# Query groups 0 and 1 loaded in 128-byte runs and transposed by VectorE, like the other 22

## The chip, the cores and the metric

One core of a Trainium2 chip runs the whole kernel. The metric is the time of one execution on the device in microseconds (us); of two kernels the one with the lower median is faster.

The engines run side by side, each through its own list of instructions in order, and wait for one another on semaphores: TensorE (PE in the profile, its weight loads PEld), VectorE (DVE), ScalarE (ACT), GpSimd (POOL) and SyncE (SP, which here only issues loads and stores). 16 DMA engines carry these out.

## What is computed

Attention of 12288 queries over 768 keys, whose result goes through two small networks. All is float32.

```python
kv_pool = kv.reshape(B, H // 4, 4, W // 4, 4, C).mean(axis=(2, 4))   # 384 x 32 pixels of 128 -> 768 keys
k = v = kv_pool.reshape(B, -1, C) @ w_sr
s = (q @ k.transpose(0, 2, 1)) / np.sqrt(C)                          # q: 12288 x 128
a = np.exp(s - s.max(-1, keepdims=True))
a /= a.sum(-1, keepdims=True) + 1e-09
x = a @ v                                                            # 12288 x 128
h = x @ w_in;  x = (np.maximum(h, 0) + alpha * np.minimum(h, 0)) @ w_out      # 128 -> 2048 -> 128
h = x @ w_in2
g = (a0 + a1*h + a2*h**2 + a3*h**3) / (1 + abs(b0)*abs(h) + abs(b1)*h**2 + 1e-06)
out = g @ w_out2                                                     # 2048 -> 128
```

Each row of q gives one row of out, so rows may be taken in any order, if the output is written back in the same.

## The kernel before

**Stages.** The kernel has three. At the start (0 to 27 us) kv is loaded in six chunks of 1 MB (each 128 rows of 8 KB), pooled 4 x 4 into 128 keys a chunk, and multiplied by w_sr to k and v. Then comes attention over 24 groups of 512 queries (to about 290 us), and then both networks over the same 24 groups (to 1530 us).

**Precision.** TensorE multiplies in a fast float32 form (fp32r). To keep precision an operand is split in two: its high part, rounded by ScalarE as it is written (k_hi, q_hi, x_hi), and its low part, the difference (k_lo, q_lo, x_lo). split_product adds three products of such parts.

**The start in the order of each engine.** SyncE issues all loads on one queue: chunk 0 in two halves, chunk 1, query group 0, chunk 2, query group 1, chunks 3 and 4, chunk 5 in two halves, w_in1, w_out1, the coefficients (L207 to L218), and then query groups 2 and later, each as soon as its buffer is free (L219 to L232). Chunk c is pooled in four units of 512 columns. VectorE sums two or three of them (pool_keys, L949), TensorE multiplies the others directly with a matrix that adds rows (pooled_transpose, L1429), and then VectorE's sums too (L1433). ScalarE copies the result out (copy_pooled_t, L463), and TensorE multiplies it by w_sr (key_chunk, L1442), after every third chunk to values as well (L1446). ScalarE and VectorE split k and v (keys_hi, keys_lo, values_hi, values_lo). TensorE takes its steps in the order pooled_transpose(0), (1), key_chunk(0), queries(0), pooled_transpose(2), key_chunk(1), queries(1), and so on (L1514 to L1525). VectorE has query_lo(0) behind pool_keys(2) and query_lo(1) behind pool_keys(3) (L1041 to L1044). ScalarE has query_hi(0) ahead of copy_pooled_t(2), and query_hi(1) ahead of copy_pooled_t(3) and keys_hi(0) (L533 to L544).

**Query groups 0 and 1.** q_in (the same memory as neg_part, 128 x 2 x 512, one buffer for even and one for odd groups) is loaded with one transfer for each: partition p takes rows 4p to 4p + 3 of its group, 2 KB in one run. Scores need queries with their 128 components over the partitions. So TensorE transposes four 128 x 128 tiles into PSUM bank Q_T (queries, L1474), ScalarE rounds from there (query_hi, L502), and VectorE subtracts (query_lo, L989).

**Query groups 2 to 23.** Four transfers load a group, one for each quarter j of the components: partitions 32j to 32j + 31, rows of 32 floats (128 bytes) each, 512 runs a transfer (L225). One 32 x 32-block transpose by VectorE (turn_query, L996) then gives q_turned with the components over the partitions; ScalarE rounds it, and GpSimd subtracts (query_lo, L264). This leaves the queries of a group in another order, and the stores undo it: four transfers of 512-byte runs for a group (L239), where groups 0 and 1 have one of 2 KB runs (L236).

**Memory.** early is a name for the memory that x_hi and x_lo take later: kv_in lies in the half of x_lo, and q_turned is before the change the last 1024 columns of it, where chunk 5 of kv lies at the start.

**Behind the start.** TensorE's first score product waits for k_lo (both halves) and q_lo (tile_scores, L1478). From then on the steps of all engines are written out by hand, without a branch.

Of the kernel before, what the change touches and what calls it, by code (L numbers as in the profile page):

```python
# [7 lines left out]
F32 = mybir.dt.float32  # L8
# [5 lines left out]
P = 128  # L14
# [20 lines left out]
def build(nc, q, kv, w_sr, w_in1, w_out1, alpha, w_in2, w_out2, coef_p, coef_q, out):  # L35
# [15 lines left out]
    q_groups = q[0].rearrange("(g p t) c -> g p (t c)", p=P, t=TILES)  # L51
    q_parts = q[0].rearrange("(g a n) (j b) -> g j a n b", a=SIDE, n=GROUP // SIDE, b=SIDE)
    out_groups = out.rearrange("(g p t) c -> g p (t c)", p=P, t=TILES)
# [3 lines left out]
    with ctx:  # L57
# [53 lines left out]
        q_turned = early[:, 2 * tokens - 2 * GROUP:].rearrange("p (b n) -> p b n", b=2)  # L111
# [10 lines left out]
        Q_T, P_T, ATT = 4, (5, 6, 4), 7  # L122
# [4 lines left out]
        for name in (  # L127

            *(f"ld_kv{c}" for c in range(CHUNKS)), "ld_kv_first", "ld_kv_rest", "spread0", "row_sums_done", "ld_wsr", "ld_in1", "ld_out1", "ld_in2", "ld_out2", "ld_al", "ld_ab", "ld_q0", "ld_q1", "ld_turned0", "ld_turned1", "q_turned", "q_lo_pool", "st_out",
# [5 lines left out]
            "qt_ready", "q_hi_done", "q_lo_done", "s_ready", "max_done", "shift_done", "exp_done", "eps_done", "inv_done",  # L135
# [15 lines left out]
        def stores(g):  # L151
            return g + (P // SIDE - 1) * max(g - 2, 0)
# [51 lines left out]
        def _(sp):  # L204

            half = UNITS // 2 * POOL_SIDE * P
            sp.dma_start(kv_in[:, 0, 0:half], kv_rows[0, 0, :, 0:half]).then_inc(s["ld_kv0"], 16)  # L207
            sp.dma_start(kv_in[:, 0, half:], kv_rows[0, 0, :, half:]).then_inc(s["ld_kv_first"], 16)
            for c in range(1, CHUNKS - 1):
                sp.dma_start(kv_in[:, c, :], kv_rows[c // 2, c % 2]).then_inc(s[f"ld_kv{c}"], 16)  # L210
                if c <= 2:
                    sp.dma_start(q_in[:, c - 1, :], q_groups[c - 1]).then_inc(s[f"ld_q{c - 1}"], 16)
# [6 lines left out]
            for g in range(GROUPS - 2):  # L219
                if g < 2:  # L220
                    sp.wait_ge(s["qt_ready"], g + 1)
                else:
                    sp.wait_ge(s["q_turned"], g - 1)
                for j in range(P // SIDE):
                    sp.dma_start(q_in[j * SIDE:(j + 1) * SIDE, g % 2, :].rearrange("a (n b) -> a n b", b=SIDE),  # L225
                                 q_parts[g + 2, j]).then_inc(s[f"ld_turned{g % 2}"], 16)
# [6 lines left out]
            for g in range(GROUPS):  # L233
                sp.wait_ge(s["y2_out_done"], g + 1)
                if g < 2:
                    sp.dma_start(out_groups[g], y_out[:]).then_inc(s["st_out"], 16)  # L236
                else:
                    for r in range(P // SIDE):
                        sp.dma_start(out_parts[g, r], y_out[r * SIDE:(r + 1) * SIDE, :].rearrange("a (t c) -> a t c", t=TILES)).then_inc(s["st_out"], 16)  # L239
# [4 lines left out]
        def _(pool):  # L244
# [16 lines left out]
            def query_lo(g):  # L261
                if group(g):
                    pool.wait_ge(s["q_hi_done"], g + 1)
                    nc.gpsimd.tensor_tensor(q_lo[:, g % 2, :], q_turned[:, g % 2, :], q_hi[:, g % 2, :].bitcast(F32),  # L264
                                            ALU.subtract).then_inc(s["q_lo_pool"], 1)
# [16 lines left out]

            for g in range(STEPS):
# [170 lines left out]
        def _(act):  # L454
# [38 lines left out]
            def query_hi(g):  # L493
                if group(g):
                    if g < 2:
                        act.wait_ge(s["qt_ready"], g + 1)
                        turned = banks[:, Q_T, :]
                    else:
                        act.wait_ge(s["q_turned"], g - 1)
                        turned = q_turned[:, g % 2, :]  # L500
                    after(act, s["s_ready"], (g - 1) * TILES)
                    nc.scalar.activation(q_hi[:, g % 2, :], turned, ACT.Copy).then_inc(s["q_hi_done"], 1)  # L502
# [436 lines left out]
        def _(dve):  # L939
# [46 lines left out]
            def query_lo(g):  # L986
                if group(g):
                    dve.wait_ge(s["q_hi_done"], g + 1)
                    nc.vector.tensor_tensor(q_lo[:, g % 2, :], banks[:, Q_T, :], q_hi[:, g % 2, :].bitcast(F32),  # L989
                                            ALU.subtract).then_inc(s["q_lo_done"], 1)  # L990

            def turn_query(g):
                if group(g):
                    dve.wait_ge(s[f"ld_turned{g % 2}"], 16 * (P // SIDE) * (g // 2))
# [850 lines left out]
```

## Time and profile before

| | us |
|---|---|
| median of 3 runs | 1532.26 (1532.25 to 1532.49) |
| profiled execution | 1533.03 |
| its span, first to last instruction | 1530.6 |

| engine | busy, us | share of the span | instructions |
|---|---|---|---|
| TensorE, matmuls | 1497.5 | 98% | 8181 |
| VectorE | 1434.1 | 94% | 2269 |
| ScalarE | 1402.4 | 92% | 2714 |
| GpSimd | 1259.0 | 82% | 1369 |

All but the first 27 us are filled almost without a gap on TensorE. These shares are means over the whole span; the start looks otherwise, and the rows below are mostly from there. A busy matmul row overlaps the next, so that 98% is no measure of TensorE at its peak. In lists by time, a row can stand for several instructions of one kind (x16), and in brackets is how long the engine had been idle before and what released it. The rows of SPq are issues, and their duration is the time SyncE spent on them, not that of the transfer.

### The profile page before, as it was taken

The page shows a single profiled execution, that of the slowest core. Times are in us where ns is not written, and L with a number is a line of the kernel's source. Part 1 is how long each engine was busy: PE and PEld are TensorE (multiplying, and loading weights), DVE is VectorE, ACT ScalarE, POOL GpSimd, SP SyncE. Part 2 cuts the span into 40 slices and gives each one's busy share as a digit, 9 for nine tenths or more (in the row PEclk, how much of TensorE's full clock was granted, in tenths as well). Part 3 has the DMA queues.
Part 4 walks back from the last instruction along what each step waited for, and adds up shares of the span by engine and source line. Part 5 has one row for each costly group of instructions (what it writes and reads, how often), then busy time and mean ns, then how long its engine had stood idle before and what let it go on. Part 6 is the DMA issues. An engine that isn't in the chain of part 4 may idle for free. (4 is left out here: it accounts for less than half of the span.)

```text
span 1530.6 us, 28132 instructions
## 1 busy us (share of the span) xinstructions
PE 1497.5 (98%) x8181; PEld 1234.5 (81%) x8181; DVE 1434.1 (94%) x2269; ACT 1402.4 (92%) x2714; POOL 1259.0 (82%) x1369
## 2 busy tenths in 40 slices
PE   7999999999999999999999999999999999999986
PEld 6989999768888888888887888887888888888865
DVE  6788888649999999999999999999999999999997
ACT  3787877669999999999999999999999999999996
POOL 1565656329999999999999999999999999999996
PEclk9999999999999999999999999999999999999998
DMA  7211210000000000000000000000000000000000
GB/s 251 55 24 27 51 27 15 1 1 1 8 8 8 1 8 8 8 1 8 8 8 8 1 8 8 8 1 8 8 7 2 7 8 8 8 1 7 8 8 8
DMA packets 62826, 24.94 MB, mean 16 GB/s; under 512 B 48448, under 2 KB 59856, under 8 KB 61904
## 3 DMA queue, kind: packets, MB, share of 16 engines
q1 hardware_dynamic: 62496, 23.08, 6.4%
q8 instruction: 64, 1.05, 0.3%
q14 instruction: 90, 0.74, 0.2%
q10 hardware_dynamic: 176, 0.07, 0.0%
HBM read 16.85 MB, written 6.29 MB: 15 GB/s over the span
## 5 line engine op out<-in xcount | busy, mean ns | idle before, releaser
L321 POOL TENSOR_TENSOR cubic<-sq,lin_p 128x512 f32<-128x512 f32 x384 | 495.5, 1290 | 75.2 <-ACT sq L596 48.3
L312 POOL TENSOR_TENSOR rational<-newton,ratio 128x512 f32<-128x512 f32 x333 | 430.1, 1292 | 30.5 <-PE banks L1616 22.2
L1616 PEld LDWEIGHTS banks<-wout,rational 128*128 128x128 f32 x3072 | 400.8, 193 | 41.9 <-issue 10.6
L1616 PE MATMUL banks<-wout,rational 128*128 128x128 f32 x3072 | 402.9, 276 | 2.5 <-POOL rational L312 1.7
L1396 PE MATMUL banks<-x_hi,win_lo 128*128 128x512 f32 x768 | 386.9, 504 | 15.6 <-DVE ratio L1105 12.3
L1398 PE MATMUL banks<-x_hi,win_hi 128*128 128x512 f32 x768 | 303.8, 396 | 0.0
L1397 PE MATMUL banks<-x_lo,win_hi 128*128 128x512 f32 x768 | 302.9, 394 | 0.0
L614 ACT ACTIVATE lin_p<-banks,ab_raw 128x512 f32<-128x512 f32 x384 | 296.5, 773 | 2.9 <-PE banks L1398 2.8
L1088 DVE SCALAR_TENSOR_TENSOR banks<-sq,abs_b,banks 128x512 f32<-128x512 f32 x384 | 286.2, 746 | 3.3 <-ACT banks L606 2.9
L1105 DVE SCALAR_TENSOR_TENSOR ratio<-banks,ab_raw,rcp 128x512 f32<-128x512 f32 x384 | 285.0, 742 | 3.0 <-POOL rational L312 0.9
L1096 DVE SCALAR_TENSOR_TENSOR banks<-banks,ab_raw,cubic 128x512 f32<-128x512 f32 x384 | 287.6, 749 | 0.0
L630 ACT ACTIVATE rcp<-log_q 128x512 f32<-128x512 f32 x384 | 278.8, 726 | 0.4
L606 ACT ACTIVATE banks<-banks 128x512 f32<-128x512 f32 x384 | 267.6, 697 | 1.5 <-DVE rational L1123 1.4
L596 ACT ACTIVATE sq<-banks 128x512 f32<-128x512 f32 x384 | 266.0, 693 | 0.7 <-PE banks L1398 0.6
L621 ACT ACTIVATE log_q<-banks 128x512 f32<-128x512 f32 x384 | 263.0, 685 | 3.6 <-DVE banks L1088 3.6
L1114 DVE SCALAR_TENSOR_TENSOR newton<-banks,rcp 128x512 f32<-128x512 f32 x333 | 224.5, 679 | 0.3
L303 POOL TENSOR_SCALAR newton<-newton 128x512 f32<-128x512 f32 x333 | 207.6, 624 | 19.8 <-DVE newton L1114 10.4
L1396 PEld LDWEIGHTS banks<-x_hi,win_lo 128*128 128x128 f32 x768 | 145.5, 189 | 92.8 <-DVE ratio L1105 23.1
L1606 PE MATMUL banks<-neg_part,wout 128*128 128x512 f32 x384 | 196.0, 592 | 0.0
L1397 PEld LDWEIGHTS banks<-x_lo,win_hi 128*128 128x128 f32 x768 | 146.1, 190 | 46.6 <-issue 31.7
L1398 PEld LDWEIGHTS banks<-x_hi,win_hi 128*128 128x128 f32 x768 | 144.7, 188 | 32.9
L1137 DVE SCALAR_TENSOR_TENSOR neg_lo<-banks,neg_hi 128x512 fp32r<-128x512 f32 x192 | 130.7, 681 | 15.7 <-ACT neg_hi L588 15.7
(96 smaller groups left out, 2269.2 us busy)
## 6 DMA issues: line engine op xcount, KB each, us to landing
neg_part<-in_q_dram SPq DMA_DIRECT2D x88, 64.0 KB, 2.6
out_dram<-y_out SPq DMA_DIRECT2D x88, 64.0 KB, 2.1
early<-in_kv_dram SPq DMA_DIRECT2D x4, 1024.0 KB, 10.8
early<-in_kv_dram SPq DMA_DIRECT2D x4, 512.0 KB, 9.6
early<-in_moe_w_in_dram SPq DMA_DIRECT2D x1, 1024.0 KB, 17.1
wout<-in_moe_w_in_dram SPq DMA_DIRECT2D x1, 1024.0 KB, 5.2
neg_part<-in_q_dram SPq DMA_DIRECT2D x2, 256.0 KB, 8.8
out_dram<-y_out SPq DMA_DIRECT2D x2, 256.0 KB, 2.2
```

The costliest lines, as they stand in the source:

```text
L312: nc.gpsimd.tensor_tensor(rational[:, m % 3, :], newton[:, m % 2, :], ratio[:, m % 2, :], ALU.mult).then_inc(s["rat_done"], 1)
L321: nc.gpsimd.tensor_tensor(cubic[:, m % 2, :], sq[:, m % 2, :], lin_p[:, m % 2, :], ALU.mult).then_inc(s["cubic_done"], 1)
L606: nc.scalar.activation(banks[:, QV[m % 2], :], banks[:, H2[m % 3], :], ACT.Abs, scale=scale_b0).then_inc(s["absb_done"], 1)
L614: nc.scalar.activation(lin_p[:, m % 2, :], banks[:, H2[m % 3], :], ACT.Identity, bias=ab_raw[:, 2:3], scale=scale_a3).then_inc(s["linp_don ...
L630: nc.scalar.activation(rcp[:, m % 2, :], log_q[:, m % 2, :], ACT.Exp, bias=float(-LN_SHIFT * np.log(2.0)), scale=-1.0).then_inc(s["rcp_don ...
L1088: nc.vector.scalar_tensor_tensor(banks[:, QV[m % 2], :], sq[:, m % 2, :], abs_b[:, 1:2], banks[:, QV[m % 2], :], ALU.mult, ALU.add).then_i ...
L1096: nc.vector.scalar_tensor_tensor(banks[:, H2[m % 3], :], banks[:, H2[m % 3], :], ab_raw[:, 1:2], cubic[:, m % 2, :], ALU.mult, ALU.add).th ...
L1105: nc.vector.scalar_tensor_tensor(ratio[:, m % 2, :], banks[:, H2[m % 3], :], ab_raw[:, 0:1], rcp[:, m % 2, :], ALU.add, ALU.mult).then_inc ...
L1396: nc.tensor.matmul(dst, w[1], x[0], start=start, stop=False)
L1397: nc.tensor.matmul(dst, w[0], x[1], start=False, stop=False)
L1398: return nc.tensor.matmul(dst, w[0], x[0], start=False, stop=stop)
L1616: last = nc.tensor.matmul(banks[:, ACC2, t * P:(t + 1) * P], rational[:, m % 3, t * P:(t + 1) * P], wout2[:, c, :], start=(c == 0 and t == ...
```

## The change

The two ways of handling queries become one. Groups 0 and 1 are loaded by four transfers each in 128-byte runs, at the place in SyncE's order where their one transfer stood; turn_query(0) and (1) stand on VectorE where query_lo(0) and (1) stood; their query_lo goes to GpSimd, ahead of its first attention step; TensorE's queries(0) and (1) go, and with them bank Q_T. Their outputs are stored by four transfers each. The buffers of groups 2 and 3 are filled once turn_query, no longer TensorE, has read groups 0 and 1. q_turned moves to the last 1024 columns of the half of x_hi, since it is now written while kv is still there. The semaphores of the two ways are merged.

```diff
-        q_turned = early[:, 2 * tokens - 2 * GROUP:].rearrange("p (b n) -> p b n", b=2)
+        q_turned = early[:, tokens - 2 * GROUP:tokens].rearrange("p (b n) -> p b n", b=2)
...
         def stores(g):
-            return g + (P // SIDE - 1) * max(g - 2, 0)
+            return g * (P // SIDE)
...
+            def load_queries(g):
+                for j in range(P // SIDE):
+                    sp.dma_start(q_in[j * SIDE:(j + 1) * SIDE, g % 2, :].rearrange("a (n b) -> a n b", b=SIDE),
+                                 q_parts[g, j]).then_inc(s[f"ld_q{g % 2}"], 16)
...
             for c in range(1, CHUNKS - 1):
                 sp.dma_start(kv_in[:, c, :], kv_rows[c // 2, c % 2]).then_inc(s[f"ld_kv{c}"], 16)
                 if c <= 2:
-                    sp.dma_start(q_in[:, c - 1, :], q_groups[c - 1]).then_inc(s[f"ld_q{c - 1}"], 16)
+                    load_queries(c - 1)
...
             for g in range(GROUPS - 2):
-                if g < 2:
-                    sp.wait_ge(s["qt_ready"], g + 1)
-                else:
-                    sp.wait_ge(s["q_turned"], g - 1)
-                for j in range(P // SIDE):
...
+                sp.wait_ge(s["q_turned"], g + 1)
+                load_queries(g + 2)
...
                 sp.wait_ge(s["y2_out_done"], g + 1)
-                if g < 2:
-                    sp.dma_start(out_groups[g], y_out[:]).then_inc(s["st_out"], 16)
-                else:
-                    for r in range(P // SIDE):
...
+                for r in range(P // SIDE):
+                    sp.dma_start(out_parts[g, r], y_out[r * SIDE:(r + 1) * SIDE, :].rearrange("a (t c) -> a t c", t=TILES)).then_inc(s["st_out"], 16)
...
+            query_lo(0)
+            query_lo(1)
             for g in range(STEPS):
...
-                    if g < 2:
-                        act.wait_ge(s["qt_ready"], g + 1)
-                        turned = banks[:, Q_T, :]
-                    else:
-                        act.wait_ge(s["q_turned"], g - 1)
-                        turned = q_turned[:, g % 2, :]
+                    act.wait_ge(s["q_turned"], g + 1)
                     after(act, s["s_ready"], (g - 1) * TILES)
-                    nc.scalar.activation(q_hi[:, g % 2, :], turned, ACT.Copy).then_inc(s["q_hi_done"], 1)
+                    nc.scalar.activation(q_hi[:, g % 2, :], q_turned[:, g % 2, :], ACT.Copy).then_inc(s["q_hi_done"], 1)
...
-            def query_lo(g):
-                if group(g):
-                    dve.wait_ge(s["q_hi_done"], g + 1)
-                    nc.vector.tensor_tensor(q_lo[:, g % 2, :], banks[:, Q_T, :], q_hi[:, g % 2, :].bitcast(F32),
-                                            ALU.subtract).then_inc(s["q_lo_done"], 1)
...
-                    dve.wait_ge(s[f"ld_turned{g % 2}"], 16 * (P // SIDE) * (g // 2))
-                    dve.wait_ge(s["s_ready"], (g - 1) * TILES)
+                    dve.wait_ge(s[f"ld_q{g % 2}"], 16 * (P // SIDE) * (g // 2 + 1))
+                    after(dve, s["s_ready"], (g - 1) * TILES)
                     nc.vector.transpose(q_turned[:, g % 2, :], q_in[:, g % 2, :]).then_inc(s["q_turned"], 1)
...
             pool_keys(2)
-            query_lo(0)
+            turn_query(0)
             pool_keys(3)
-            query_lo(1)
+            turn_query(1)
...
-            def queries(g):
-                if group(g):
-                    pe.wait_ge(s[f"ld_q{g % 2}"], 16 * (g // 2 + 1))
-                    after(pe, s["q_lo_done"], g)
-                    for t in range(TILES):
-                        last = nc.tensor.transpose(banks[:, Q_T, t * P:(t + 1) * P], q_in[:, g % 2, t * P:(t + 1) * P], ident[:])
-                    last.then_inc(s["qt_ready"], 1)
...
             key_chunk(0)
-            queries(0)
             pooled_transpose(2)
             key_chunk(1)
-            queries(1)
```

## Rows read from the trace of the kernel before

**Rows 1.** Busy time by stretch: stretch, length, PE, PEld, DVE, ACT, POOL, clock, DMA, GB/s.
```profile
100.00:200.00 100.00, 100.00 (x599) 90.16 (x599) 86.20 (x153) 78.32 (x151) 59.73 (x120) 1.00 0.19 35
```

**Rows 2.** Timeline of TensorE: start, duration, line, out<-in, count, idle time before.
```profile
4.47 3.41 PE L1429 MATMUL banks<-early 128*128 128x128 f32 x16 [4.47 <-DMA early<-in_kv_dram]
...
9.21 2.05 PE L1429 MATMUL banks<-early 128*128 128x128 f32 x16 [0.72 <-DMA early<-in_kv_dram]
...
11.56 0.39 PE L1442 MATMUL banks<-wout,early 128*128 128x128 f32 x2
...
18.75 0.49 PE L1433 MATMUL banks<-early 128*128 128x128 f32 x2 [0.45 <-DVE early L949]
...
19.97 1.95 PE L1429 MATMUL banks<-early 128*128 128x128 f32 x16
...
22.43 1.95 PE L1429 MATMUL banks<-early 128*128 128x128 f32 x16
...
26.85 0.44 PE L1396 MATMUL banks<-k_hi,q_lo 128*128 128x384 f32 x1 [0.50 <-DVE k_lo L956]
```

**Rows 3.** Timeline of VectorE in the start.
```profile
9.19 1.99 DVE L949 TENSOR_REDUCE early<-early 128x128 f32<-128x512 f32 x2 [2.46 <-DMA early<-in_kv_dram]
...
12.35 2.91 DVE L949 TENSOR_REDUCE early<-early 128x128 f32<-128x512 f32 x3 [1.09 <-DMA early<-in_kv_dram]
...
15.77 2.92 DVE L949 TENSOR_REDUCE early<-early 128x128 f32<-128x512 f32 x3
```

**Rows 4.** Timeline of SyncE's issues in the start.
```profile
0.73 0.39 SPq L207 DMA_DIRECT2D early<-in_kv_dram  x1
...
2.59 0.43 SPq L210 DMA_DIRECT2D early<-in_kv_dram  x1
...
3.56 0.94 SPq L210 DMA_DIRECT2D early<-in_kv_dram  x2
...
7.54 15.33 SPq L217 DMA_DIRECT2D ab_raw<-in_moe_a_dram  x1
```

**Rows 5.** Busy time by stretch again: the last two columns are DMA share, GB/s.
```profile
1.00:2.00 1.00, 0.00 (x0) 0.00 (x0) 0.18 (x1) 1.00 (x1) 0.55 (x3) 1.00 0.24 53
...
23.00:24.00 1.00, 1.00 (x12) 1.00 (x11) 1.00 (x2) 0.06 (x1) 0.00 (x0) 1.00 1.03 299
24.00:25.00 1.00, 1.00 (x10) 0.85 (x8) 0.05 (x1) 0.14 (x1) 0.00 (x0) 1.00 0.74 186
...
26.00:31.00 5.00, 3.94 (x26) 3.45 (x25) 2.92 (x5) 1.84 (x5) 0.52 (x3) 1.00 0.64 100
...
46.00:52.00 6.00, 6.00 (x38) 5.52 (x37) 4.47 (x8) 4.64 (x10) 3.22 (x7) 1.00 0.29 46
```

**Rows 6.** DMA issues from 2.5 to 2.8 us; lines L210 and L225: landings, issues.
```profile
early<-in_kv_dram SPq DMA_DIRECT2D x1, 1024.0 KB, 9.7
...
DMA to landing us min/median/max: 7.5/10.8/13.9
...
L225 SPq DMA_DIRECT2D neg_part<-in_q_dram x8: 560/627/875, 46.3 to 59.5; - x8
```

**Rows 7.** DMA engines' busy tenths in 40 equal slices of 46.3 to 50 us.
```profile
DMA  0000000000000004799600642021049999932594
```

**Rows 8.** Instructions by line: ns min/median/max, first and last start in us.
```profile
L996 DVE STREAM_TRANSPOSE early<-neg_part x22: 691/702/711, 35.6 to 265.9; 128x512 f32<-128x512 f32 x22
...
L989 DVE TENSOR_TENSOR q_lo<-banks,q_hi x2: 676/678/679, 15.2 to 18.6; 128x512 fp32r<-128x512 f32 x2
...
L502 ACT ACTIVATE q_hi<-early x22: 617/623/629, 37.6 to 269.6; 128x512 fp32r<-128x512 f32 x22
...
L264 POOL TENSOR_TENSOR q_lo<-early,q_hi x22: 1289/1299/1309, 43.3 to 275.0; 128x512 fp32r<-128x512 f32 x22
```

**Rows 9.** Timeline: GpSimd's first shift in the attention phase.
```profile
29.24 0.19 POOL L258 TENSOR_TENSOR exp_shift<-neg_max,scale_col 128x1 f32<-128x1 f32 x1 [27.45 <-DVE neg_max L1010]
```

**Rows 10.** Stores of groups 0 and 1, by line.
```profile
L236 SPq DMA_DIRECT2D out_dram<-y_out x2: 332/343/354, 390.3 to 440.0; - x2
```

## Predicting the time of the changed kernel

> **What bounds the kernel now.** I read three things, in this order. First, the busy time of the engines in one stretch of the attention phase: from 100 to 200 us TensorE is never idle [rows 1]. Nothing there can swallow a delay from further up front: what the kernel loses before its first score matmul, it ends later by. Second, the start, engine by engine: where the first score matmul comes from. It starts at 26.85 us, behind the second half of k_lo [rows 2]; from there back the chain runs over TensorE's pooling of chunks 5 and 4 (16 matmuls each, 22.43 and 19.97) to the last pooling matmul of chunk 3 at 18.75, which waited for VectorE [rows 2]. VectorE sums chunk 3 from 15.77 and chunk 2 from 12.35, and chunk 2's sums waited for their load; so did those of chunk 1 at 9.19 [rows 3]. Third, the queue of loads: SyncE issues them one behind the other on one queue [rows 4], and from 2 us on the 16 DMA engines are full, at 23 us still with a share of 1.03 [rows 5]. So up to chunk 3 the start goes at the pace of that queue, then of VectorE and TensorE. The loads of queries 0 and 1 stand in the queue ahead of chunks 2 and 3. That is the place to read.
>
> The landings: chunk 2 was issued at 2.59 and took 9.7 us, so 12.3; chunk 3 at 3.56. Of the four loads of L210 the shortest took 7.5 (chunk 1), the median is 10.8 and the longest 13.9 (chunk 4), so chunk 3's is 2 x 10.8 - 9.7 = 11.9, landing at 15.5, and chunk 4's, issued about 0.5 later, lands at 18.0 [rows 4, 6]. Chunk 4 follows chunk 3 by 2.5 us, a chunk's own time; chunk 2 follows chunk 1 (9.19, when its waiting sums start [rows 3]) by 3.1. The difference, 0.6 us, is a query group in 2 KB runs.
>
> **Queries 0 and 1 as eight loads of 128-byte runs.** Queries 2 and later are loaded that way already. Two groups took a share of 0.64 of the engines for 5 us, 1.6 us each; another, alone, 0.29 of 6 us, 1.7 [rows 5]. I take 1.6: in place of 0.6 that is +1.0 for chunk 2 and +2.0 for chunk 3. It is 12.5 ns for each of 128 runs on an engine. (The Trainium skill, DMA: Bandwidth & Descriptors, Why small descriptors are slow, gives a fixed cost of about 3 cycles a packet; by it a 128-byte run would be 7 cycles at 850 MHz, 8.2 ns, a group 1.05 us as an estimate, and chunk 3 only 0.9 late before any gap. The trace has a third more than that, and I go by the trace.)
>
> **The queue has an end.** The small load of L217 was issued at 7.54 and held SyncE for 15.33 us [rows 4], until 22.87. What then stood in the queue was the rest of w_out1's load in 512-byte runs: 0.13 us at some 299 GB/s, a microsecond at 299 and one at 186 [rows 5], about 0.52 MB, or 64 runs for each of 16 engines. Earlier, ten loads of 8 rows for each engine were issued by 6 us, when little more than chunk 0 had left (chunk 1 landed at 9.19), so some 60 stood there without such a hold. So I read the queue's room as 64 to 72 runs per engine. A quarter of a query group is 32 runs per engine and takes 0.63 us to issue [rows 6]. Chunks 0 and 1 are 24 rows and two quarters 64 runs; the third waits until chunk 1 has nearly left, and the fourth is issued at about the moment T at which chunk 1's data ends. Chunk 2 is issued 0.63 later, and its data starts 1.0 us behind that (the first load: issued 0.73, data from about 1.75, a share of 0.24 of the second microsecond [rows 4, 5]) to 1.3 (a query load issued at 46.27, data from the 15th of 40 slices of 3.7 us [rows 7]), plus up to 0.3 for what is not yet pushed: T + 1.65 to T + 2.25 or so. Without a gap it would be T + 1.6. I take T + 2.05, a gap of 0.45 in which the engines starve. The same again ahead of chunk 3, whose quarters can be queued only 64 runs deep behind chunk 2. So chunk 2 lands 1.45 later and chunk 3, 4 and 5 land 2.9 later; bounds 2.0 (no gaps) and 3.7 (0.85 each).
>
> **What of it counts.** Chunk 3 lay landed for 0.3 us (15.46 to 15.77) while VectorE still worked on chunk 2 [rows 3]; this cover goes. Chunk 2's sums run 13.8 to 16.7, and chunk 3 now arrives at 18.4: chunk 3's sums start at 18.4 instead of 15.77, +2.6. Behind it everything keeps its distance: chunk 4 lands at 20.9 and TensorE wants it at 22.6, and chunk 5, one load of 2.5 us behind it, 2.5 us later.
>
> **VectorE.** Two transposes of 0.70 us for two subtractions of 0.68 [rows 8], +0.04. The first lies where VectorE now waits for chunk 3, the second ahead of chunk 4's sums, which end before TensorE has done its 16 matmuls of that chunk: 0. As the source is loaded ahead of the chunk summed just before, neither waits for a load. **TensorE** loses 8 transposes, which lay where it would next wait for VectorE's sums: 0. **ScalarE** reads SBUF instead of PSUM, 0.62 us a group as for the later groups [rows 8]. Its queue is in order: query_hi(0) now waits for the transpose behind chunk 2's sums, so copy_pooled_t(2), behind it in the queue, comes 1.4 us after those sums instead of 0.6. Its reader key_chunk(2) comes behind chunk 3's pooling: hidden. The same with copy_pooled_t(3) and keys_hi(0), which would be done some 2.1 us after chunk 3's sums; keys_lo(0) is at 2.6. That is the tightest cover, 0.5 us, and without it VectorE would be late by what is missing. **GpSimd** takes two subtractions of 1.30 us [rows 8]; it sat idle for 27.45 us until its first shift [rows 9], and the scores want them only at 29: 0. **SyncE** is freed about 3 us later, at 25.8 instead of 22.87; query group 2, issued from 27 on, lands by 32, and its transpose was at 35.6 [rows 8] and moves to 38: 0. w_in1 and w_out1, which stand between chunk 5 and query group 2 in the queue, move by 3 as well, and so do their readers, TensorE's steps behind the first scores: 0. **Stores** of groups 0 and 1: eight issues for two; the next write of y_out comes some 50 us later, since the two stores began at 390.3 and 440.0 [rows 10]: 0. q_turned lies elsewhere, at the same size and the same 0.70: 0.
>
> **Sum.** 2.9 - 0.3 = 2.6 us. The profiled execution, 1533.03 (span 1530.6), would become 1535.6; the median is 0.77 below it, and the time goes by that: 1532.26 + 2.6 = 1534.9.
>
> **Rivals.** (a) No gaps: SyncE keeps the queue fed. 2.05 - 0.3 = 1.75, giving 1534.0. For it: 64 queued runs last 0.8 us, longer than an issue of 0.63. Against: the first data takes 1.0 to 1.3. (b) Full gaps of 0.85: 3.75 - 0.3 = 3.45, giving 1535.7, slower. This is the forecast's mechanism with its other end: the queue is refilled so late that each chunk starts 2.5 us after its forerunner ended. It decides from a landing of chunk 3 at 18.9 on (3.4 late). For it: the one query load whose start the trace shows apart had 1.3 us to its first data. (c) TensorE's clock. The granted column reads 1.00 throughout, yet the first 16 pooling matmuls took 3.41 us against 1.95 for chunk 5's [rows 2], as at 1.2 instead of 2.4 GHz. Its idle stretch ahead of chunk 1 was 0.72 us; now it sits idle for 1.9 us ahead of chunk 2 (from 11.95, where key_chunk(0) ends [rows 2]) and 1 ahead of chunk 3. If the clock fell and stayed down for chunks 4 and 5, their 16 matmuls would take 3.41 instead of 1.95 us: +2.9 more, 1537.8. (The Trainium skill, TensorE: Matmul & The Clock Gate, says the clock halves after idle time and returns after sustained work; by that rule it is a question of how idle the start becomes.) Against it: TensorE waits for VectorE again and again up to 18.75, and chunk 5's matmuls are at full speed all the same. (d) It is all hidden, because something other than the loads bounds chunk 3: 1532.3. Against: chunk 2's sums waited 1.09 us for their load [rows 3]. (e) Some gain by GpSimd or TensorE of over 3 us: no row shows where.
>
> **How the numbers follow.** Forecast 0.42, (a) 0.18, (b) 0.27, (c) 0.06, (d) 0.05, (e) 0.02. 0.2% is 3.06 us, about what a measurement of this kernel can tell from no change. Slower is (b), (c) and 0.03 of the forecast's upper edge, 0.36; faster is (e), 0.02; within is the rest, 0.62. The range leaves out (c), (d) and (e), 0.13, and the outer edges of the others: 1533.5 to 1536.6.
>
> **What would show it.** SyncE's issues of the third or fourth query quarter held for microseconds; chunk 2 landing near 13.8 and chunk 3 near 18.4; the first score matmul at 29.4 and from there on a constant shift. Wrong, if chunk 3 lands within 1 us of 15.5, if VectorE waits for keys_hi(0), or if the shift changes after 30 us.

## The result and the profile after

| | before | changed kernel |
|---|---|---|
| median of 12 runs each, us | 1532.53 (1529.18 to 1535.29) | 1536.09 (1534.6 to 1537.27) |
| ratio | | 1.0019, 95% interval 1.0011 to 1.0026 |
| profiled execution, us | 1533.03 | 1535.4 |
| its span, us | 1530.6 | 1533.6 |
| first score matmul, us | 26.85 | 29.77 |

The change makes the kernel a little slower: 1.7 to 4.0 us. The ratio lies at the edge of the 0.2% that I had called no change. In the trace it is there when the first score matmul starts: 29.77 us against 26.85. SyncE's issues in the changed kernel (they answer to [rows 4]; a duration is how long SyncE was held):

```profile
2.11 3.60 SPq L206 DMA_DIRECT2D neg_part<-in_q_dram  x4
5.75 2.96 SPq L213 DMA_DIRECT2D early<-in_kv_dram  x1
8.75 2.87 SPq L206 DMA_DIRECT2D neg_part<-in_q_dram  x4
11.66 2.69 SPq L213 DMA_DIRECT2D early<-in_kv_dram  x2
```

Chunk 2 was issued at 2.59 before; now SyncE comes to it at 5.75 and is held there until 8.71. VectorE (beside [rows 3]), from chunk 1's sums on:

```profile
9.52 2.00 DVE L941 TENSOR_REDUCE early<-early 128x128 f32<-128x512 f32 x2 [2.53 <-DMA early<-in_kv_dram]
...
14.62 2.92 DVE L941 TENSOR_REDUCE early<-early 128x128 f32<-128x512 f32 x3 [3.02 <-DMA early<-in_kv_dram]
17.45 0.70 DVE L982 STREAM_TRANSPOSE early<-neg_part 128x512 f32<-128x512 f32 x1
18.68 2.93 DVE L941 TENSOR_REDUCE early<-early 128x128 f32<-128x512 f32 x3 [0.53 <-DMA early<-in_kv_dram]
21.53 0.70 DVE L982 STREAM_TRANSPOSE early<-neg_part 128x512 f32<-128x512 f32 x1
```

The idle time ahead of chunk 2 grew from 1.09 to 3.02 us, and chunk 3, which had waited for VectorE, is now waited for. TensorE (beside [rows 2]):

```profile
14.64 2.08 PE L1415 MATMUL banks<-early 128*128 128x128 f32 x8 [2.36 <-DMA early<-in_kv_dram]
...
25.34 1.95 PE L1415 MATMUL banks<-early 128*128 128x128 f32 x16
...
29.77 0.44 PE L1382 MATMUL banks<-k_hi,q_lo 128*128 128x384 f32 x1 [0.50 <-DVE k_lo L948]
```

From the start of chunk 3's sums to the first score matmul it is 11.09 us, against 11.08 before: nothing between the two costs anything. And the shift stays, within 0.3 us. Write of y_out for group 0 (390 us) and group 21 (1432 us), first before, then after:

```profile
389.63 0.68 DVE L1152 TENSOR_SCALAR y_out<-banks 128x512 f32<-128x512 f32 x1
...
1432.49 0.68 DVE L1152 TENSOR_SCALAR y_out<-banks 128x512 f32<-128x512 f32 x1
```

```profile
392.55 0.68 DVE L1138 TENSOR_SCALAR y_out<-banks 128x512 f32<-128x512 f32 x1
...
1435.08 0.68 DVE L1138 TENSOR_SCALAR y_out<-banks 128x512 f32<-128x512 f32 x1
```

The shift is 2.92 us at the first score matmul and at group 0, and 2.59 at group 21. Behind 1450 us the granted clock of TensorE dips in every trace, in another pattern each time (mean from 1450 to 1529 us: 0.89 before, 0.89 after), which spreads the ends: from the last but two outputs to the last it took 93.0 us before, 93.1 after, and between 92.9 and 95.0 in the kernels below. So for effects of a microsecond I read the start of a trace rather than its end.

### The profile page after: what moved, and what is told of

Read it like the earlier page. It is cut to its first block and busy times, and to the rows that moved or that the text cites. A ratio compares the mean times of both kernels' runs of the same rounds, so it can differ in the third digit from the quotient of the medians.

```text
span 1533.6 us, 28129 instructions
## 1 busy us (share of the span) xinstructions
PE 1497.3 (98%) x8173; PEld 1234.8 (81%) x8173; DVE 1434.2 (94%) x2269; ACT 1401.3 (91%) x2714; POOL 1262.3 (82%) x1371
## 3 DMA queue, kind: packets, MB, share of 16 engines
q8 instruction: 64, 1.05, 0.3%
```

## The experiments

**How they are compared.** Chunk 1's sums start between 8.26 and 9.75 us in the traces, also in kernels that issue the same up to there. What follows is steadier, so the last column counts from there. Each ratio is taken against runs of the kernel before on the same chip.

| kernel | chunk 1's sums start | chunk 2 behind chunk 1 | chunk 1's sums to first score matmul | ratio to before (95%) |
|---|---|---|---|---|
| before | 9.19 | 3.16 | 17.66 | 1 |
| changed | 9.52 | 5.10 | 20.25 | 1.0019 (1.0011 to 1.0026) |
| changed, again | 9.75 | 5.08 | 20.51 | 1.0020 (1.0011 to 1.0029) |
| changed, long runs | 8.41 | 3.21 | 17.71 | 0.9998 (0.9989 to 1.0007) |
| before, 128-byte runs, one transfer | 8.85 | 4.89 | 20.49 | 1.0023 (1.0012 to 1.0034) |
| before, 256-byte runs, one transfer | 8.74 | 3.74 | 18.44 | 1.0000 (0.9991 to 1.0010) |
| before, four narrow transfers | 9.67 | 4.07 | 18.58 | 1.0014 (1.0005 to 1.0023) |
| before, four wide transfers | 8.81 | 3.52 | 18.06 | 1.0003 (0.9993 to 1.0013) |
| changed, two quarters a chunk | 8.37 | 3.73 | 17.94 | 1.0003 (0.9994 to 1.0013) |
| changed, queries late (three times) | 8.26, 8.91, 9.10 | 2.48 to 2.50 | 16.39 each | 0.9998, 0.9995, 0.9993 |
| before, queries late | 8.29 | 2.48 | 16.84 | 0.9994 (0.9984 to 1.0003) |

**Undo the loads alone.** Values are in the wrong places; the work is the same.

```diff
                 if c <= 2:
-                    load_queries(c - 1)
+                    sp.dma_start(q_in[:, c - 1, :], q_groups[c - 1]).then_inc(s[f"ld_q{c - 1}"], 16)
```

> The changed kernel with one part undone: query groups 0 and 1 come again in one transfer each of 2 KB runs (their values then lie in the wrong places, the work is the same); transposes by VectorE, low parts on GpSimd and four stores a group stay. In the changed kernel the first score matmul starts at 29.77 us instead of 26.85, and I put all of it down to the loads. Theory (the loads in short runs are the whole cost): chunk 2's sums start near 12.3, chunk 3's near 15.9, the first score matmul at 26.9 (26.7 to 27.2), and the time is within 0.8 us of before. Rival (VectorE's transposes, ScalarE's order or GpSimd's low parts cost too): the first score matmul stays at 27.9 or later, a third or more of the 2.9 us, although chunk 2 lands as before.

The first score matmul came at 26.12, 17.71 behind chunk 1's sums, as before (17.66); the median was 1531.90 against 1532.57. VectorE's transposes, ScalarE's order, GpSimd's low parts, the removed transposes of TensorE and the eight stores together cost nothing that can be seen in the start (0.05 us), and the interval of the ratio leaves them at most 1.1 us. The loads are the cost of the change.

**Short runs without the four issues.**

```diff
-                    sp.dma_start(q_in[:, c - 1, :], q_groups[c - 1]).then_inc(s[f"ld_q{c - 1}"], 16)
+                    sp.dma_start(q_in[:, c - 1, :].rearrange("p (n b) -> p n b", b=SIDE),
+                                 q_short[c - 1][:, :, 0:SIDE]).then_inc(s[f"ld_q{c - 1}"], 16)
```

> The kernel before with one part of the change: groups 0 and 1 in 128-byte runs, but each in a single transfer over all 128 partitions (it reads 16 rows of 32 components a partition, so these queries are wrong values; nothing else differs). 128 runs for each engine as in the change, one issue in place of four. Theory A (the engines starve between SyncE's issues; a run takes 12.5 ns): no gap is left, a group takes 1.6 us, chunk 2 is 1.0 and chunk 3 2.0 late, the first score matmul comes at 28.6, and the time is 1.7 above before. Theory B (runs that stand in a queue take longer, some 19 ns, and the number of issues does not matter): a group takes 2.5 us as in the changed kernel, chunk 3 lands 3.2 late, the first score matmul at 29.7, and the time is 2.9 above before.

Theory A misses: with one issue for each group, chunk 2 still follows by 4.89 us and 20.49 remain, as in the changed kernel. Theory B has the sum right (chunk 3 3.2 us later behind chunk 1) and its reason wrong. The DMA engines in quarters of a microsecond (last columns: granted clock, DMA share, GB/s), first in the changed kernel, then in the kernel before:

```profile
8.25:8.50 0.25, 0.25 (x4) 0.24 (x3) 0.00 (x0) 0.00 (x0) 0.00 (x0) 1.00 1.37 208
...
9.00:9.25 0.25, 0.00 (x0) 0.00 (x0) 0.00 (x0) 0.00 (x0) 0.00 (x0) 1.00 0.45 59
9.25:9.50 0.25, 0.00 (x0) 0.00 (x0) 0.00 (x0) 0.00 (x0) 0.00 (x0) 1.00 1.78 254
9.50:9.75 0.25, 0.21 (x1) 0.21 (x2) 0.23 (x1) 0.00 (x0) 0.00 (x0) 1.00 0.83 138
9.75:10.00 0.25, 0.25 (x4) 0.25 (x4) 0.25 (x1) 0.00 (x0) 0.00 (x0) 1.00 0.66 131
...
11.00:11.25 0.25, 0.25 (x5) 0.25 (x4) 0.25 (x1) 0.00 (x0) 0.00 (x0) 1.00 0.62 262
```

```profile
9.75:10.00 0.25, 0.25 (x5) 0.25 (x4) 0.25 (x1) 0.00 (x0) 0.00 (x0) 1.00 0.85 360
10.00:10.25 0.25, 0.25 (x5) 0.25 (x4) 0.25 (x2) 0.00 (x0) 0.00 (x0) 1.00 0.93 393
```

While short runs stand in the queue they move at 208 GB/s, so a group would take 262 KB / 208 = 1.26 us, less than my 1.6. Then, around 9 us, the engines run dry, and chunk 2's 8 KB rows come in slowly: its load moves at 131 to 262 GB/s up to 11.25, where chunks move at 411 in the kernel before (9 to 11 us). Why they come in slowly the runs do not show. The single transfer does the same, at 66 to 75 GB/s behind a quarter with 347:

```profile
8.25:8.50 0.25, 0.25 (x3) 0.25 (x2) 0.00 (x0) 0.00 (x0) 0.00 (x0) 1.00 1.31 206
...
9.00:9.25 0.25, 0.25 (x3) 0.20 (x2) 0.25 (x1) 0.12 (x1) 0.00 (x0) 1.00 0.29 44
9.25:9.50 0.25, 0.25 (x3) 0.25 (x3) 0.25 (x1) 0.16 (x1) 0.00 (x0) 1.00 2.54 347
9.50:9.75 0.25, 0.25 (x5) 0.25 (x4) 0.25 (x1) 0.00 (x0) 0.00 (x0) 1.00 0.28 75
9.75:10.00 0.25, 0.25 (x5) 0.25 (x4) 0.25 (x2) 0.00 (x0) 0.00 (x0) 1.00 0.23 66
```

and its SyncE was held at chunk 2:

```profile
2.12 0.71 SPq L213 DMA_DIRECT2D neg_part<-in_q_dram  x1
2.87 5.79 SPq L211 DMA_DIRECT2D early<-in_kv_dram  x1
```

So it is the gap of my prediction, but it does not come from the pace of SyncE's issues: chunk 2's issue is held behind 128 runs, whether they came by four issues or by one, and returns when most of them have gone.

**Half as many runs.** The same edit with rows of 64 components and 8 rows a partition.

> The same experiment as the single transfer of 128-byte runs, at another size: groups 0 and 1 each in one transfer of 256-byte runs over 128 partitions, 64 runs for each engine in place of 128 (it reads 8 rows of 64 components a partition, so these queries are wrong values). With 128-byte runs chunk 2's sums started 4.89 us behind chunk 1's and chunk 3's 4.54 behind that, where 2 KB runs have 3.1 each: 1.8 and 1.4 more. Theory C (the price goes by the number of runs, each 12.5 to 17 ns): half the runs, half the price, 0.6 to 0.9 more for each group; chunk 2 follows chunk 1 by 3.8 to 4.0 and the first score matmul is 1.0 to 1.5 us later than before. Theory D (most of the price is that the queue is full and chunk 2 can be queued only when little is left): 64 runs and the rows ahead of them still find room, or nearly, no hold of a microsecond on SyncE ahead of chunk 2, and under 0.4 more for each group; the first score matmul comes within 0.5 us of before.

Between the theories: chunk 2 followed by 3.74 us, 0.6 more than with 2 KB runs, and 18.44 us were left, 0.8 more than before. But 128 runs had cost 1.7 for chunk 2, nearly three times that of 64. SyncE was held for 1.56 us at chunk 2 in place of 5.79. A price by the run alone would have doubled; the rest goes with the longer hold.

**Four transfers, long runs.**

```diff
+                    for j in range(P // SIDE):
+                        sp.dma_start(q_in[j * SIDE:(j + 1) * SIDE, c - 1, :],
+                                     q_groups[c - 1, j * SIDE:(j + 1) * SIDE]).then_inc(s[f"ld_q{c - 1}"], 16)
```

> The kernel before with the other part of the change: groups 0 and 1 in four transfers each of 32 partitions, but still in 2 KB runs (2 for each engine and transfer). Theories A and B both: the engines have 24 rows of chunks 0 and 1 ahead, the queue is never full of these, chunk 3 lands within 0.3 us of before, the first score matmul at 26.9, time within 0.5 us of before. Rival (each transfer has a fixed price on the queue, or 32 partitions at a time load slower): six more transfers make chunk 3 more than 1 us late and the time more than 0.7 us higher.

A miss for both theories and for me; what came is the rival that I had named beside them. Chunk 2 followed by 4.07 us instead of 3.16, and the ratio is 1.0014, with no short run and no full queue (the issue of chunk 2 took 0.42 us). The engines were busy all the while at a lower rate, first here, then in the kernel before:

```profile
8.00:10.00 2.00, 1.49 (x9) 1.27 (x9) 0.33 (x1) 0.28 (x1) 0.00 (x0) 1.00 1.07 301
```

```profile
8.00:10.00 2.00, 1.28 (x11) 1.06 (x11) 0.81 (x1) 0.28 (x1) 0.00 (x0) 1.00 1.07 440
```

In short runs the same cut adds little: chunk 2 follows by 5.10 and 5.08 us with four narrow transfers and by 4.89 with one wide one.

**Four transfers, cut by columns instead.**

```diff
+                    for t in range(TILES):
+                        sp.dma_start(q_in[:, c - 1, t * P:(t + 1) * P],
+                                     q_groups[c - 1][:, t * P:(t + 1) * P]).then_inc(s[f"ld_q{c - 1}"], 16)
```

> The kernel before with each of groups 0 and 1 in four transfers, as in the experiment with four transfers of 2 KB runs, but cut by columns instead of partitions: each transfer covers all 128 partitions, in 512-byte runs (8 for each engine). With four transfers of 32 partitions chunk 2 followed chunk 1 by 4.07 us instead of 3.1 to 3.2, and chunk 1 itself, which stands ahead of them, landed at 9.67 (9.52 and 9.75 in the two traces of the changed kernel), against 8.26 to 9.19 in the nine traces without four narrow transfers behind it. Theory N (what costs is the narrowness: transfers of 32 partitions load slower and hold up the end of the chunk ahead of them): here chunk 2 follows chunk 1 by 3.1 to 3.4, chunk 1's sums start before 9.3, and from there to the first score matmul it is 17.6 to 17.9. Theory M (the number of transfers costs): chunk 2 follows by 3.8 or more, chunk 1 starts after 9.4, and it is 18.3 or more.

Close to N: chunk 2 follows by 3.52 (N had 3.1 to 3.4), chunk 1 starts at 8.81, and it is 18.06, between the two, with runs of 512 bytes as part of it. So more than half of the price of four transfers (0.55 of the 0.91 us for chunk 2) is that each covers only 32 partitions. Chunk 1's start fits too: it is 9.52, 9.75 and 9.67 in the three traces with four narrow transfers behind it, and 8.26 to 9.19 in the ten others that load the queries on SyncE's queue. So the load right ahead of four narrow transfers seems to land later, by some 0.9 us on the mean (9.65 against 8.7 for the ten). In the three traces with queries late, below, chunk 4 is that load, and lands 2.7, 3.2 and 3.2 us behind chunk 3, against 2.5 in the kernel before with late loads. All this rests on a comparison of traces, not on one edit, and two narrow transfers did not do it: the variant with two quarters behind each chunk has them behind chunk 1 and starts at 8.37.

**The queries on ScalarE's queue.**

```diff
+            for g in range(2):
+                for j in range(P // SIDE):
+                    act.dma_start(q_in[j * SIDE:(j + 1) * SIDE, g, :].rearrange("a (n b) -> a n b", b=SIDE),
+                                  q_parts[g, j]).then_inc(s[f"ld_q{g}"], 16)
```

> The changed kernel with one thing moved: the eight query loads of groups 0 and 1 are issued by ScalarE on its own queue, behind its two small loads, and the chunks of kv follow one another on SyncE's queue. Both queues are served by the same 16 DMA engines. Theory D (the full queue ahead of the chunks is what costs): SyncE is never held ahead of chunks 2 to 5, only the engines' time for the runs is left, 1.0 us a group more than 2 KB runs, and chunk 3's sums start by 17.5 at the latest (18.68 in the changed kernel, 15.77 before); the first score matmul at 28.6 or earlier. Theory C' (what costs is the engines' time in runs and in small transfers, whichever queue they are in): chunk 3 starts at 18.3 or later and the first score matmul at 29.4 or later; chunks 0 and 1 land later than in the changed kernel, since the queries now go beside them. A side effect in both: ScalarE itself is held by its issues, so that its first copy of pooled keys may come late.

1545.76 us against 1532.62, ratio 1.0084, and the first score matmul at 40.67. That is past the 29.4 of theory C', but not for its reason: the chunks ran as theory D had it, SyncE was not held ahead of them, and chunk 2 followed chunk 1 by 2.62 us. What cost was the side effect that I had named in passing, ScalarE's hold, and with it the queries, which hardly moved beside the chunks:

```profile
1.68 24.14 ACTq L456 DMA_DIRECT2D neg_part<-in_q_dram  x8
```

```profile
11.34 2.87 DVE L943 TENSOR_REDUCE early<-early 128x128 f32<-128x512 f32 x3 [0.56 <-DMA early<-in_kv_dram]
26.79 0.71 DVE L984 STREAM_TRANSPOSE early<-neg_part 128x512 f32<-128x512 f32 x1 [12.58 <-DMA neg_part<-in_q_dram]
```

```profile
26.30 0.77 PE L1430 MATMUL banks<-wout,early 128*128 128x128 f32 x2 [14.82 <-ACT wout L462]
```

ScalarE was held in its issues for 24.14 us, VectorE waited 12.58 us for group 0, and TensorE 14.82 us for the first copy by ScalarE, so either alone would have cost about as much. The packets of the two queues from 6 to 20 us (packets, MB, share of 16 engines; q1 has the large rows, q10 the short runs):

```profile
q1 hardware_dynamic: 905, 5.58, 97.6%
q10 hardware_dynamic: 896, 0.11, 5.4%
```

The engines took about one short run for each large row: 896 runs in 14 us on 16 engines are one in 250 ns, against one in 9.8 ns in the changed kernel. (The Trainium skill, DMA: Bandwidth & Descriptors, Queues, rings and completion order, says that each engine goes round between the queues that have work, a packet at a time. The 905 and 896 packets agree with it, one run of 128 bytes for each large row.)

**Two quarters behind each chunk.**

```diff
-                if c <= 2:
-                    load_queries(c - 1)
+                load_queries((c - 1) // 2, (0, 1) if c % 2 else (2, 3))
```

> The changed kernel with the same eight short-run transfers spread: two quarters (64 runs for each engine) behind each of the chunks 1 to 4 in place of four behind chunks 1 and 2; the transposes one chunk later on VectorE, ScalarE's order to match. In the traces so far chunk 1's landing moves by up to 1.4 us between kernels that do not differ before it, so I compare from the start of chunk 1's sums to the first score matmul: 17.66 us before, 20.25 in the changed kernel, 18.44 with 256-byte runs. Theory D (the full queue costs beside the runs themselves: 64 runs fit in it, so the next chunk is queued in time and a pair costs its runs, 0.8 us): each chunk follows the last by 3.3 us, chunk 3 comes 0.4 later than before relative to chunk 1, and 17.7 to 18.0 us remain of the 20.25. Theory C (only the runs cost, 16 to 17 ns each wherever they stand): each chunk follows by 3.6, and it is 18.3 or more.

17.94 us, in D's range; the ratio is 1.0003. But chunk 2 follows chunk 1 by 3.73, which is C's mark (3.6) and not D's (3.3). The same eight transfers of the same runs cost 0.3 us in place of 2.6. Here the engines do not run dry behind a pair of quarters; the rate is back at once:

```profile
8.25:8.50 0.25, 0.25 (x3) 0.25 (x3) 0.13 (x1) 0.00 (x0) 0.00 (x0) 1.00 1.28 454
8.50:8.75 0.25, 0.25 (x3) 0.18 (x1) 0.25 (x1) 0.00 (x0) 0.00 (x0) 1.00 0.85 296
8.75:9.00 0.25, 0.25 (x3) 0.09 (x1) 0.25 (x1) 0.00 (x0) 0.00 (x0) 1.00 0.85 328
9.00:9.25 0.25, 0.25 (x2) 0.21 (x2) 0.25 (x1) 0.24 (x1) 0.00 (x0) 1.00 1.28 524
```

SyncE was held here too, though:

```profile
5.90 2.30 SPq L213 DMA_DIRECT2D early<-in_kv_dram  x1
```

That is the issue of chunk 3. It returned at 8.20, while chunk 2's rows were still coming in, and no gap followed. So a hold seems to cost only where nothing long is left to move meanwhile.

Two things are mixed in this variant: no more than 64 runs of queries stand between two chunks, and the second half of the runs stands behind chunk 3, where VectorE has work. The first is seen at chunk 2, which follows by 3.73: a pair costs 1.2 us over a chunk's own 2.5, where 0.8 was expected. How much each of the two is worth is not shown.

**The changed kernel again.**

> The changed kernel itself once more, beside the variants on one chip. From the start of chunk 1's sums to the first score matmul it took 20.25 us against 17.66, 2.6 more. If that shift is its whole effect, it is 20.1 to 20.5 again and the ratio to before is 1.0012 to 1.0024, 1.8 to 3.7 us; if the 3.6 us between the medians of the first comparison were real in full, it would be above 1.0020 and something behind the start would have to be slower.

20.51 us and a ratio of 1.0020: 1536.30 against 1533.08. It agrees with the first comparison.

**Queries late.** Group 0 between chunks 4 and 5, group 1 behind chunk 5; the transposes and ScalarE's rounding moved to match.

```diff
                 sp.dma_start(kv_in[:, c, :], kv_rows[c // 2, c % 2]).then_inc(s[f"ld_kv{c}"], 16)
-                if c <= 2:
-                    load_queries(c - 1)
+            load_queries(0)
...
+            load_queries(1)
             sp.dma_start(raw_in[0], w_in1).then_inc(s["ld_in1"], 16)
...
             pool_keys(4)
+            turn_query(0)
             keys_lo(0)
             pool_keys(5)
             values_lo(0)
             keys_lo(1)
+            turn_query(1)
```

> The changed kernel with the query loads moved back in the queue: group 0 between chunks 4 and 5, group 1 behind chunk 5; the transpose of group 0 behind VectorE's sums of chunk 4, that of group 1 behind the last keys_lo; ScalarE's rounding moved to match. If the cost is only that the short runs stand ahead of chunks 2 and 3, then chunk 2 lands 0.6 and chunk 3 1.2 us earlier than in the kernel before (11.7 and 14.3), VectorE's own sums set the pace from chunk 2 on, and the first score matmul comes 1.1 us earlier than before, at 25.7 (25.4 to 26.2): 4 us below the changed kernel and 1.1 below the one before, a median near 1531.4. Rival: chunk 5, now some 2.2 us behind chunk 4 plus its own time, becomes late for TensorE, or group 0's low part does; then the first score matmul comes at 27 to 28, slower than before.

> The variant with late query loads once more, since its 11 runs did not agree with its trace: there the first score matmul came at 24.65 instead of 26.85, the output of group 0 2.0 and that of group 21 2.35 us earlier than before, and 1.8 of it was gone at the end, where TensorE's granted clock falls to half now and then from 1475 us on, in another pattern in every trace. Theory (that end is drawn anew in each run and has nothing to do with the change): over both sets of runs the median is 1 to 2.3 us below before, near 1531. Rival (a start earlier by 2 us ends no earlier, because the end absorbs it): the median stays within 0.5 us of before although output 21 is again 2 us earlier.

> The variant with late query loads on the same chip as the changed kernel and as the other variant. From chunk 1's sums to the first score matmul it took 16.39 us both times, 1.27 less than before. If nothing behind the start takes it back, the median is 1.0 to 1.5 us below before and 3.5 to 4.2 below the changed kernel, and the first score matmul follows chunk 1's sums by 16.4 again. Rival: the end takes it back, and the median is within 0.5 us of before.

In the start it does what was expected, and a little more, three times: 16.39 us, 1.27 less than before and 3.9 to 4.1 less than the changed kernel. VectorE sums chunks 2 to 4 without a stop (second trace):

```profile
11.41 7.64 DVE L941 TENSOR_REDUCE early<-early 128x128 f32<-128x512 f32 x8 [0.43 <-DMA early<-in_kv_dram]
18.97 0.70 DVE L982 STREAM_TRANSPOSE early<-neg_part 128x512 f32<-128x512 f32 x1
```

The medians are 1532.37, 1531.64 and 1531.98, which is 0.2, 1.0 and 1.1 below before beside them. Each ratio is below 1 and each interval includes it (0.9989 to 1.0007, 0.9986 to 1.0004, 0.9984 to 1.0002). The first median missed the 1531.4 expected; the second lies at the lower edge of what was expected (1 to 2.3 below), the third inside (1.0 to 1.5 below). Against the changed kernel on the same chip it is 4.3 us faster (1531.98 and 1536.30). That it beats the kernel before is likely, and not shown.

**The kernel before with late loads.** Group 0 and 1 in 2 KB runs between chunks 4 and 5; TensorE's transposes of group 0 ahead of chunk 5's pooling.

> The kernel before with the same idea and without the change: groups 0 and 1 in 2 KB runs as before, their loads between chunks 4 and 5, TensorE's transposes of group 0 ahead of chunk 5's pooling and of group 1 behind the last values, ScalarE's and VectorE's halves to match. Chunks 2 and 3 come 0.6 and 1.2 us earlier; VectorE's sums set the pace as in the variant with late short runs. If four transposes on TensorE's path cost their 0.5 us, the first score matmul follows chunk 1's sums by 16.9 us, against 16.4 there: then the way of the change is worth 0.5 us once the loads stand late. Rival: they fit in a wait of TensorE and it is 16.4 here too; or group 0's low part is late and it is 17.2 or more.

16.84 us: the four transposes cost their 0.45 us on TensorE's path, as the first theory said. By time the two late variants cannot be told apart (ratios 0.9993 and 0.9994). So VectorE's way of transposing is worth half a microsecond in the trace of the start, but only once the loads stand where short runs hurt nobody.

## Why the prediction was right

**The place and the mechanism** were right: the loads of groups 0 and 1 delay chunk 3, all else is hidden, and the shift is carried on nearly unchanged (2.92 us at group 0, 2.59 at group 21). The long-run experiment shows the second part, the outputs of groups 0 and 21 the third. SyncE's hold came one issue later than I had it: the four quarters of group 0 took 3.60 us together, 1.1 more than at 0.63 each, and it was chunk 2's own issue that stood for 2.96 us. So SyncE had issued all 128 runs of the group by 5.71 us, before any of them moved, where a room of 64 to 72 runs would have stopped it at the third quarter. What the hold does to chunk 2, which cannot be queued until little but short runs is left, is as I had reasoned.

**The sum.** Predicted: chunk 3 2.9 us later, 2.6 of it at the first score matmul. Measured from chunk 1 on: 2.59 and 2.85 at the first score matmul. Chunk 3 follows chunk 1 by 9.16 and 9.44 us (18.68 and 19.19), where its landing followed by 6.27 before [rows 3, 6], 2.9 and 3.2 more. The terms were off and cancelled, so that the closeness of the sum is in part luck:

- A group at 1.6 us: queued runs need 1.26. The rows I took were of loads that were issued one after another onto an empty queue. The estimate from the Trainium skill (DMA: Bandwidth & Descriptors, Why small descriptors are slow), 1.05 us, was nearer than I gave it credit for; the trace has 9.8 ns a run in place of its 8.2.
- The gap at 0.45 each: with chunk spacings of 5.10 and 4.06, a chunk's 2.5 and 1.26 for the runs, 1.3 is left ahead of chunk 2 and 0.3 ahead of chunk 3, 1.6 together (1.9 in the second trace), where I had 0.9. I had taken it for a start that comes late. It is a start that comes late and then rows that come in slowly, at 131 to 262 GB/s. How it divides between the two chunks the landings need not show: chunk 3's rows start as slowly as chunk 2's (first trace, below), and chunk 2 has four narrow transfers behind it and may itself have landed late, as chunk 1 seems to.
- The reason for the gap at SyncE's four issues: it is the full queue, with one issue as with four.
- Not in the sum at all: narrow transfers. Chunk 1 seems to land some 0.9 us later with four of them behind it. The changed kernel's first score matmuls, 29.77 and 30.26, are 3.5 above the mean of the two traces with 2 KB runs in one transfer (26.85 and 26.12), and the medians differ by 3.6 and 3.2. That would account for most of what 1536.09 is above the 1534.9 predicted, 1.2 us, of which 0.3 is the higher median of the kernel before. But the single wide transfer of short runs, whose first score matmul came at 29.34, 2.9 above those two traces, has a median 3.5 above before as well. The medians cannot tell 2.9 from 3.5 us (the intervals of the two ratios are 2.3 and 3.4 us wide), so what made up the last microsecond stays open.

The DMA engines ahead of chunk 3 in the first trace of the changed kernel (last columns: granted clock, DMA share, GB/s):

```profile
14.25:14.50 0.25, 0.00 (x0) 0.00 (x0) 0.00 (x0) 0.00 (x0) 0.00 (x0) 1.00 0.48 73
14.50:14.75 0.25, 0.11 (x1) 0.11 (x1) 0.13 (x1) 0.00 (x0) 0.00 (x0) 0.84 2.71 386
14.75:15.00 0.25, 0.25 (x1) 0.25 (x2) 0.25 (x1) 0.00 (x0) 0.00 (x0) 0.50 0.58 98
15.00:15.25 0.25, 0.25 (x3) 0.25 (x3) 0.25 (x1) 0.00 (x0) 0.00 (x0) 0.50 0.57 131
```

**The covers.** Every one held. keys_hi(0), the tightest, was done at 23.44 and its keys_lo started at 24.08: 0.64 us where I had 0.5. GpSimd's subtractions ran at 18.90 and 22.98, ScalarE's second copy 1.2 us behind chunk 2's sums.

**The rivals.** (b), full gaps, has its mark in chunk 3's landing at 18.68 and 19.19, around its threshold of 18.9. Its gaps, 1.7 us together, are nearer to the 1.6 and 1.9 measured than my 0.9; its 1.6 us for a group is too long. Behind chunk 1's sums chunk 3 came 2.9 and 3.2 us later, where it had 3.7 and I 2.9. (a) is out. (c) came in half: TensorE's granted clock did fall to 0.50 behind the idle time ahead of chunk 2.

```profile
15.00:16.00 1.00, 1.00 (x6) 1.00 (x6) 1.00 (x2) 0.00 (x0) 0.00 (x0) 0.50 0.68 213
...
18.00:19.00 1.00, 0.82 (x6) 0.63 (x6) 0.47 (x2) 0.79 (x2) 0.10 (x1) 0.96 0.97 410
```

It was back before chunk 4, whose 16 matmuls took their 1.95 us. It cost nothing: it was over before chunk 3's sums began at 18.68, and those waited for their load. In the single wide transfer of short runs it read 0.50 up to 19 us, past the start of chunk 3's sums at 18.28, and from there to the first score matmul it still took 11.06 us. In the second trace of the changed kernel it did not fall at all, behind 2.34 us of idle time against 2.36. (The Trainium skill, TensorE: Matmul & The Clock Gate, What's actually happening, has the clock fall after idle time; the first trace agrees, and the second shows that a like idle time need not do it.) (d) and (e) are out.

## What to carry to other kernels

A load in many short runs can hold the issue behind it, so it costs little by itself and much by what is queued behind it: put it behind the last large load that somebody waits for, or spread it between large ones. Here 128 runs for each engine ahead of a chunk made it 1.7 to 1.9 us later and 64 runs 0.6, each over one 2 KB-run transfer. Price a load by the spacing of the loads around it when the queue is full, not by its own time on an empty queue. And before a change adds work to a busy start, look for the engine that idles there later: in the traces of the start the same eight transfers cost 2.6 us, 0.3 us or less than nothing by where they stood.

## What the hardware showed that I had not expected

- Transfers over 32 partitions load more slowly than those over 128, with 2 KB runs and an unfilled queue: 301 GB/s from 8 to 10 us instead of 440, chunk 2 following at 4.07 instead of 3.16 us, and with four of them the load ahead seems to land late as well.
- No single room of the queue fits all holds. The one of 15.33 us [rows 4] gave 64 to 72 runs for each engine, yet a transfer of 128 runs was issued in 0.71 us, and the issue behind it was held for 5.79. After so many short runs the next large load comes in at 131 to 262 GB/s for about 2 us, where chunks move at 411.
- Short runs on a second queue beside large rows on the first nearly stand still, at about one run for each large row (896 and 905 packets in 14 us): eight transfers of 64 KB held their issuer for 24.14 us.
